# Token rows and gate sums of the channel mixing from y's high and low halves, behind the first receptance product

## Chip, cores and metric

One Trainium2 chip, one core. The time is the device time of the core in microseconds; the kernel before takes 770.95 us, the median of three runs (769.91 to 771.16).

## What is computed

Three layers one behind the other: attention under a block mask, channel mixing (RWKV's), and a mixture of eight experts in which a gate may hold the expert of the token before. The change lies in the second layer and in the hand-over to the third.

```python
def _moe_ref(x, mu_k, mu_r, w_k, w_v, w_r):          # x: 4 x 576 x 512
    x_prev = np.concatenate([np.zeros((B, 1, D)), x[:, :-1, :]], axis=1)
    xk = mu_k * x + (1.0 - mu_k) * x_prev
    xr = mu_r * x + (1.0 - mu_r) * x_prev
    k = np.maximum(xk @ w_k, 0.0)                    # 1024 wide
    v = k * k @ w_v
    r = 1.0 / (1.0 + np.exp(-(xr @ w_r)))
    return r * v                                     # called y below

def _moe2_ref(x, w_gate, w_local, w1, w2):           # x = y, token by token
    logits = x @ w_gate                              # 8 gates
    local_gate = 1.0 / (1.0 + np.exp(-(x @ w_local)))
    # the expert is argmax(logits) where local_gate < 0.5, else that of the token before
    # out = softmax(logits)[e] * (relu(x @ w1[e]) @ w2[e])
```

## The kernel before

All heavy products are done in two halves: an operand a is kept as its rounded part (type float32r, "hi") and the remainder ("lo"), and a product is hi*hi + hi*lo + lo*hi, three one-pass matmuls (`product`, lines 839 to 843). The high half is made by ACT with a copy, the low half by DVE with a subtraction.

The channel mixing takes the 2304 tokens in six steps of 384 columns (`NSTEP`, `NT`), features on the partitions. In step s the tensor engine (`mlp_step`, line 911) does eight K products of 12 matmuls (`k_done`), four receptance products R of 12 (`r_done`), then for s > 0 the rows of the step before (`rows_chunk(s - 1, c)`, four chunks), and four V products of 24 (`v_done`). V products use two PSUM banks in turn, so the third one waits for the first y: `wait(pe, y_done, DC * s + d - 1)`.

The rows: the third layer gathers tokens, so y (features on partitions, tile `yT`) is turned to token rows in DRAM, and the gate sums are made with it. `rows_chunk` multiplies 128 tokens of a chunk of yT, as the stationary operand, with 137 columns: the identity and beside it the nine gate columns of that chunk (tile `idw`). Both are plain float32. There are 12 such matmuls in a step. In the last step the rows of chunks 0 to 2 stand behind the V products 1 to 3, those of chunk 3 behind the loop (line 966).

ACT (`mlp_act`, line 1247) makes relu and the square's high half behind each K product, an exponential for each R product into tile `sig`, the high halves of the next step's inputs, and copies the rows from PSUM to `ytok` (`copy_rows`, three copies, after the logits are read). After the last step come the high halves of the first expert's weights (`split_we_hi`) and of its first token tile (`x_hi`).

DVE (`mlp_vec`, line 1536) makes the square and its low half for each K product, then for each exponential an addition and a reciprocal (lines 1562 and 1564), the low halves of the next step's inputs at the second and fourth, the gate sums of the step before (`read_logits`, three operations), and the four y (line 1578). In step 4 it routes the first twelve groups of tokens between the y (`pre_route`); PE takes part with small matmuls inside the V products (`between`). In step 5 it makes low halves of expert weights between the y (`first_weights`); after y 3 come the last rows, the last gate sums and the rest of the routing. SP stores `ytok` after the third copy and loads the first expert's weights in step 5; POOL gathers the token tiles.

Each engine runs its instructions in the order written; they wait for each other by semaphores with counts. PE's waits are written out by hand.

Of the kernel before, what the change touches and what calls it, by code (L numbers as in the profile page):

```python
# [5 lines left out]
F32 = mybir.dt.float32  # L6
# [4 lines left out]
ALU = mybir.AluOpType  # L11
# [5 lines left out]
def attention_moe_program(nc, qkT, v, mu_k, mu_r, w_k, w_v, w_r, w_gate9, w1, w2, out):  # L17
# [36 lines left out]
    with ExitStack() as ctx:  # L54
# [94 lines left out]
        yT = place("work", "yT", [P, DC, NT])  # L149
        ytok = place("work", "ytok", [P, GPS, DM])  # L150
        early_w2_raw = top["work"]
# [132 lines left out]
        def third_at(j):  # L284
# [8 lines left out]
                 "xm_split k_done relu_done ksq_done ksq_is_hi ksq_split r_done rexp_done sig_done v_done y_done "  # L293
# [5 lines left out]
         xm_is_hi, xm_split, k_done, relu_done, ksq_done, ksq_is_hi, ksq_split, r_done, rexp_done, sig_done, v_done, y_done,  # L299
# [63 lines left out]
        RW = P + GATE  # L363
# [326 lines left out]
        def _(pe):  # L690
# [133 lines left out]
            def rows_chunk(s, c):  # L824

                pe.wait_ge(y_done, DC * s + c + 1)
                at = PAD if c % 2 else PAD - GATE
                rhs = idw[:, c // 2, at:at + P + GATE]
                for g in range(GPS):
                    bank, col = (KB + g, c * RW) if c < DC - 1 else (KB + GPS, g * RW)  # L830
                    last = mm(ps[:, bank, col:col + RW], yT[:, c, g * G:(g + 1) * G], rhs, start=True, stop=True)  # L831
                return last
# [78 lines left out]
            def mlp_step(s):  # L911
# [27 lines left out]
                if s:  # L939
                    rows_free(s - 1)  # L940
                    for c in range(DC):
                        last = rows_chunk(s - 1, c)
                    last.then_inc(rows_done, 1)
# [205 lines left out]
        def _(act):  # L1149
# [97 lines left out]
            def mlp_act(s):  # L1247

                for f in range(FC):
                    k = FC * s + f  # L1250
                    act.wait_ge(k_done, k + 1)
                    wait(act, ksq_done, k - 1)
                    wait(act, ksq_is_hi, k - 1)
                    nc.scalar.activation(relu_k[:, f % 2, :], ps[:, KB + f % 2, 0:NT], ACT.Relu).then_inc(relu_done, 1)  # L1254
                    if s == 0:
                        xm_first(f // DC, 1 - f // DC, f % DC)
                    elif s + 1 < NSTEP:
                        xm_first(s + 1, f // DC, f % DC)
                    if s == 0 and f == DC:
                        xm_hi(0, 1)  # L1260
                    act.wait_ge(relu_done, k + 1)
                    nc.scalar.activation(ksq_hi[:, f, :], relu_k[:, f % 2, :], ACT.Square).then_inc(ksq_is_hi, 1)
                if s + 1 < NSTEP:
                    xm_hi(s + 1, 0)
                wait(act, y_done, DC * s)
                if s == 0:
                    act.wait_ge(norm_done, NHEAD)
                for d in range(DC):
                    act.wait_ge(r_done, DC * s + d + 1)
                    exp(sig[:, d, :], ps[:, RB + d % 2, 0:NT], scale=-1.0).then_inc(rexp_done, 1)  # L1270
                if s == 0:
                    for c in range(DC):
                        xm_first(1, 1, c)
                if s + 1 < NSTEP:
                    xm_hi(s + 1, 1)
                if s:
                    copy_rows(s - 1)

            def copy_rows(s):

                act.wait_ge(logits_read, s + 1)
                wait(act, y_stored, 16 * s)
                groups = ps[:, KB:KB + GPS, :]
                nc.scalar.activation(ytok[:, :, 0:2 * P], groups[:, :, GATE:GATE + 2 * P], ACT.Copy).then_inc(ytok_done, 1)
                nc.scalar.activation(ytok[:, :, 2 * P:3 * P], groups[:, :, 2 * RW + GATE:3 * RW],
                                     ACT.Copy).then_inc(ytok_done, 1)
# [33 lines left out]
            for s in range(NSTEP):  # L1320
                mlp_act(s)
            split_we_hi(0, 0)
            act.wait_ge(r_done, DC * NSTEP)
            act.wait_ge(ksq_split, FC * NSTEP)
            split_we_hi(0, 1)
            x_hi(0)
            copy_rows(NSTEP - 1)
# [41 lines left out]
        def _(dve):  # L1369
# [165 lines left out]

            def mlp_vec(s):
# [52 lines left out]
            def read_logits(s):  # L1589
# [5 lines left out]
                vec.tensor_reduce(lg, groups[:, :, 2 * RW - GATE:2 * RW + GATE].rearrange("p g (a e) -> p g e a", a=2),  # L1595
                                  AX.X, ALU.add).then_inc(lg_sums, 1)
                dve.wait_ge(lg_sums, 2 * s + 1)
# [317 lines left out]
```

## Time and profile before

| | |
|---|---|
| median of 3 runs | 770.95 us (769.91 to 771.16) |
| the profiled execution | 772.05 us, of it 770.3 in the span of instructions |
| mean granted clock of TensorE in it | 0.991 |
| attention | up to about 205 us of the span |
| channel mixing, steps 0 to 5 | 205 to 474 us, a step of 384 tokens about 45 us |
| routing and expert tiles | 474 to 770 us |

The profile is one execution. A row of the trace's timeline has a start from the beginning of the span, a duration, the engine, the source line, the operation with out<-in, the shapes and a count; behind it in brackets the idle time of the engine before it and what ended that. Successive matmuls overlap, so their cost is the distance of their starts, not their duration.

### The profile page before, as it was taken

How to read it: one execution, taken by the hardware profiler on the slowest of the kernel's cores; microseconds unless marked ns; L12 is line 12 of the kernel's file. 1: busy time of each engine (PE TensorE's matmuls, PEld its weight loads, DVE VectorE, ACT ScalarE, POOL GpSimd, SP SyncE). 2: the span in 40 equal slices, each digit the busy share in tenths (PEclk: the TensorE clock that was granted, in tenths of full speed). 3: DMA queues.
4: the chain of work that ended last, by engine and by line, in shares of the span. 5: the costliest groups of instructions: out<-in, count | busy, mean ns of one | idle time of the engine just before them, and what ended most of it. 6: DMA issues, size and time to landing. Idle time of an engine off the chain costs nothing.

```text
span 770.3 us, 13475 instructions
## 1 busy us (share of the span) xinstructions
PE 741.0 (96%) x4054; PEld 661.7 (86%) x4055; DVE 494.1 (64%) x905; ACT 357.5 (46%) x702; POOL 182.9 (24%) x215
## 2 busy tenths in 40 slices
PE   5999999998999999999999999999999999999994
PEld 4888888886989999999999998788888788888882
DVE  8899999996586856859487797622223745453261
ACT  4687877875652606244251432222124644353250
POOL 3345455453200000000020000223323232323231
PEclk9999999998999999999999999999999999999997
DMA  5667676551000010100101071167110176441000
GB/s 158 212 202 224 195 228 190 165 159 43 24 1 1 0 42 1 42 1 1 42 1 43 3 270 42 43 246 274 41 32 27 41 257 235 143 144 40 20 22 8
DMA packets 43063, 74.41 MB, mean 97 GB/s; under 512 B 10061, under 2 KB 20470, under 8 KB 43012
## 3 DMA queue, kind: packets, MB, share of 16 engines
q1 hardware_dynamic: 38676, 64.30, 25.3%
q0 software_dynamic: 4336, 9.47, 3.6%
q8 instruction: 27, 0.44, 0.2%
q14 instruction: 24, 0.20, 0.1%
HBM read 65.31 MB, written 10.57 MB: 99 GB/s over the span
## 4 chain that ended last, share of the span: by engine, by line
PE 83%; DVE 10%; issue 2%; ACT 2%; DMA 1%; ACTq 0%; POOL 0%; POOLq 0%; DVEq 0%
PE ps L841 20%; PE ps L842 20%; PE ps L843 20%; PE ps L779 3%; PE ps L707 2%; PE ps L999 2%; PE ps L733 2%; PE ps L732 2%; PE ps L831 2%; DVE negm L1380 2%; PE ps L710 2%; PE ps L774 1%; DVE sig L1564 1%; PE ps L753 1%; PE ps L908 1%
## 5 line engine op out<-in xcount | busy, mean ns | idle before, releaser
L841 PE MATMUL ps<-we_hi,hT_hi 128*128 (+1 forms) x176 | 73.4, 417 | 2.1 <-DVE o_sb L1856 1.4
L841 PE MATMUL ps<-we_hi,xgT_hi 128*128 (+1 forms) x176 | 70.6, 401 | 0.2 <-DVE xgT_lo L1755 0.2
L1317 ACT ACTIVATE hT_hi<-ps 128x512 fp32r<-128x512 f32 x44 | 26.1, 597 | 94.5 <-PE ps L999 49.4
L842 PE MATMUL ps<-we_lo,xgT_hi 128*128 (+1 forms) x176 | 69.7, 396 | 0.0
L843 PE MATMUL ps<-we_hi,xgT_lo 128*128 (+1 forms) x176 | 69.7, 396 | 0.0
L842 PE MATMUL ps<-we_lo,hT_hi 128*128 (+1 forms) x176 | 69.5, 395 | 0.0
L843 PE MATMUL ps<-we_hi,hT_lo 128*128 (+1 forms) x176 | 69.4, 394 | 0.0
L1151 ACT ACTIVATE pT<-ps 128x256 f32<-128x256 f32 (+2 forms) x192 | 63.1, 388 | 9.3 <-PE ps L733 8.9
L841 PE MATMUL ps<-xm_k_hi,wk_hi 128*128 128x384 f32 x192 | 65.2, 339 | 2.0 <-DVE ksq L1543 1.7
L841 PE MATMUL ps<-ksq_hi,wv_hi 128*128 128x384 f32 x192 | 66.0, 344 | 0.9 <-DVE yT L1578 0.9
L531 POOL TENSOR_TENSOR hi<-qk_raw,hi 64x576 fp32r<-64x576 f32 x32 | 45.2, 1412 | 85.8 <-DVE aug L1407 85.8
L842 PE MATMUL ps<-ksq_lo,wv_hi 128*128 128x384 f32 x192 | 64.9, 338 | 0.0
L843 PE MATMUL ps<-ksq_hi,wv_lo 128*128 128x384 f32 x192 | 64.9, 338 | 0.0
L843 PE MATMUL ps<-xm_k_hi,wk_lo 128*128 128x384 f32 x192 | 64.6, 336 | 0.0
L842 PE MATMUL ps<-xm_k_lo,wk_hi 128*128 128x384 f32 x192 | 64.5, 336 | 0.0
L1749 DVE TENSOR_TENSOR we_lo<-we_raw,we_hi (+1 forms) x48 | 55.6, 1221 | 11.3 <-ACT we_hi L1296 11.3
L1564 DVE RECIPROCAL sig<-sig 128x384 f32<-128x384 f32 x24 | 61.3, 2553 | 0.8
L1254 ACT ACTIVATE relu_k<-ps 128x384 f32<-128x384 f32 x48 | 23.6, 491 | 81.2 <-PE ps L843 81.2
L1762 DVE TENSOR_TENSOR hT_lo<-ps,hT_hi 128x512 fp32r<-128x512 f32 x44 | 30.0, 686 | 45.2 <-ACT hT_hi L1317 45.2
L1380 DVE TENSOR_REDUCE negm<-ps 128x1 fp32r<-128x128 f32 (+3 forms) x128 | 56.2, 479 | 2.1 <-PE ps L707 0.3
L732 PE MATMUL ps<-hi 128*128 128x256 f32 (+2 forms) x192 | 53.7, 297 | 2.3 <-ACT pT L1151 2.2
L628 POOL DMA_INDIRECT out<-o_sb,idx_out x21 | 21.5, 1023 | 139.4 <-DVE o_sb L1856 139.4
(277 smaller groups left out, 1835.4 us busy)
## 6 DMA issues: line engine op xcount, KB each, us to landing
we_raw<-w SPq DMA_DIRECT2D x12, 2048.0 KB, 11.8
qk_raw<-qkT SPq DMA_DIRECT2D x32, 576.0 KB, 3.9
v_sb<-v SPq DMA_DIRECT2D x16, 320.0 KB, 4.9
inv<-inv_scratch SPq DMA_DIRECT2D x32, 144.0 KB, 4.3
y_scratch<-ytok SPq DMA_DIRECT2D x6, 768.0 KB, 3.5
wk_raw<-w_k SPq DMA_DIRECT2D x8, 256.0 KB, 4.5
wv_raw<-w_v SPq DMA_DIRECT2D x8, 256.0 KB, 4.9
wr_raw<-w_r SPq DMA_DIRECT2D x4, 256.0 KB, 4.8
```

The costliest lines, as they stand in the source:

```text
L531: nc.gpsimd.tensor_tensor(hi[i % NBUF][DH:P, KEY, :], qk_raw[DH:P, i % 2, 1, :], hi[i % NBUF][DH:P, KEY, :].bitcast(F32), ALU.subtract).th ...
L732: mm(dst, hi[b][:, KEY, keys], hi[b][:, Q, q0:q1], start=True, stop=False)
L841: mm(dst, a_hi, b_hi, start=(k == 0), stop=False)
L842: mm(dst, a_hi, b_lo, start=False, stop=False)
L843: return mm(dst, a_lo, b_hi, start=False, stop=(k == n - 1))
L1151: return nc.scalar.activation(dst, src, ACT.Exp, **kw)
L1254: nc.scalar.activation(relu_k[:, f % 2, :], ps[:, KB + f % 2, 0:NT], ACT.Relu).then_inc(relu_done, 1)
L1317: nc.scalar.activation(hT_hi[:, half * FC // 2:(half + 1) * FC // 2, :].rearrange("p f t -> p (f t)"), ps[:, 3 + half, :], ACT.Copy).then_ ...
L1380: last = vec.tensor_reduce(negm[:, i % 2, t:t + 1], ps[:, bank, col:col + keys], AX.X, ALU.max, negate=True)
L1564: vec.reciprocal(sig[:, d, :], sig[:, d, :]).then_inc(sig_done, 1)
L1749: vec.tensor_tensor(we_lo[part][:, third], we_raw[part][:, third], we_hi[part][:, bass.ds(slot_at(j) + k * EPIECE, EPIECE)].bitcast(F32), ...
L1762: vec.tensor_tensor(hT_lo[:, fs, :].rearrange("p f t -> p (f t)"), ps[:, 3 + half, :], hT_hi[:, fs, :].rearrange("p f t -> p (f t)").bitca ...
```

## The change

- New tiles: `y_hi` and `y_lo`, of yT's size. `y_hi` lies where `sig` lies, `y_lo` where `yT` lies. `idr` holds the products' other operand in float32r: for each of two pairs of chunks the identity, with the high and the low part of nine gate columns on either side of it. It is made once, by five DVE operations after the last y of step 0 (`rows_rhs`).
- After each y (except chunk 3 of the last step) ACT makes `y_hi` (`cast_y`) and DVE `y_lo` (`split_y`), DVE waiting for ACT. In step 0 DVE makes all four low halves after y 3. In ACT's order the four casts of a step stand behind `copy_rows` of the step before; those of the last step stand before, between and behind the casts of expert weights.
- `rows_chunk` does two one-pass matmuls of 146 columns, y_hi and then y_lo by the same `idr`, added up in PSUM, in place of one float32 matmul of 137. Chunk 3 of the last step stays as it was.
- PE does the rows block of step s - 1 behind the first R product of step s, no longer behind the fourth.
- ACT waits for `rows_done` before the first exponential of a step.
- `read_logits` adds four gate parts in its first operation instead of two, and has five operations in place of three (four in the last step).

```diff
+        y_hi = nc.alloc_sbuf_tensor_at("y_hi", [P, DC, NT], R32, offset=top["work"] - 2 * 4 * DC * NT)
+        y_lo = nc.alloc_sbuf_tensor_at("y_lo", [P, DC, NT], R32, offset=top["work"] - 4 * DC * NT)
         ytok = place("work", "ytok", [P, GPS, DM])
+        idr = place("work", "idr", [P, 2, P + 4 * GATE], R32)
...
-        RW = P + GATE
+        RW = P + 2 * GATE
...
             def rows_chunk(s, c):
 
-                pe.wait_ge(y_done, DC * s + c + 1)
-                at = PAD if c % 2 else PAD - GATE
-                rhs = idw[:, c // 2, at:at + P + GATE]
+                if (s, c) == (NSTEP - 1, DC - 1):
+                    pe.wait_ge(y_done, DC * NSTEP)
+                    for g in range(GPS):
+                        last = mm(ps[:, KB + GPS, g * RW:g * RW + P + GATE], yT[:, c, g * G:(g + 1) * G],
+                                  idw[:, 1, PAD:PAD + P + GATE], start=True, stop=True)
+                    return last
+                pe.wait_ge(y_split, DC * s + c + 1)
+                at = 2 * GATE * (c % 2)
+                rhs = idr[:, c // 2, at:at + RW]
                 for g in range(GPS):
                     bank, col = (KB + g, c * RW) if c < DC - 1 else (KB + GPS, g * RW)
-                    last = mm(ps[:, bank, col:col + RW], yT[:, c, g * G:(g + 1) * G], rhs, start=True, stop=True)
+                    tokens = slice(g * G, (g + 1) * G)
+                    mm(ps[:, bank, col:col + RW], y_hi[:, c, tokens], rhs, start=True, stop=False)
+                    last = mm(ps[:, bank, col:col + RW], y_lo[:, c, tokens], rhs, start=False, stop=True)
                 return last
...
                     last.then_inc(r_done, 1)
-                if s:
-                    rows_free(s - 1)
-                    for c in range(DC):
-                        last = rows_chunk(s - 1, c)
-                    last.then_inc(rows_done, 1)
+                    if s and d == 0:
+                        pe.wait_ge(rhs_split, 2)
+                        rows_free(s - 1)
+                        for c in range(DC):
+                            last = rows_chunk(s - 1, c)
+                        last.then_inc(rows_done, 1)
...
                     act.wait_ge(norm_done, NHEAD)
+                wait(act, rows_done, s)
                 for d in range(DC):
                     act.wait_ge(r_done, DC * s + d + 1)
...
                 if s:
                     copy_rows(s - 1)
+                if s + 1 < NSTEP:
+                    for d in range(DC):
+                        cast_y(s, d)
+
+            def cast_y(s, d):
+
+                act.wait_ge(y_done, DC * s + d + 1)
+                nc.scalar.activation(y_hi[:, d, :], yT[:, d, :], ACT.Copy).then_inc(y_is_hi, 1)
...
             for s in range(NSTEP):
                 mlp_act(s)
+            cast_y(NSTEP - 1, 0)
             split_we_hi(0, 0)
+            cast_y(NSTEP - 1, 1)
             act.wait_ge(r_done, DC * NSTEP)
             act.wait_ge(ksq_split, FC * NSTEP)
             split_we_hi(0, 1)
             x_hi(0)
+            cast_y(NSTEP - 1, 2)
             copy_rows(NSTEP - 1)
...
+            def split_y(s, d):
+
+                dve.wait_ge(y_is_hi, DC * s + d + 1)
+                vec.tensor_tensor(y_lo[:, d, :], yT[:, d, :], y_hi[:, d, :].bitcast(F32), ALU.subtract).then_inc(y_split, 1)
+
+            def rows_rhs():
+
+                gates = [(idw[:, :, PAD - GATE:PAD], 0), (idw[:, :, PAD + P:PAD + P + GATE], 2 * GATE + P)]
+                vec.tensor_copy(idr[:, :, 2 * GATE:2 * GATE + P], idw[:, :, PAD:PAD + P])
+                for given, at in gates:
+                    vec.tensor_copy(idr[:, :, at:at + GATE], given).then_inc(rhs_hi, 1)
+                dve.wait_ge(rhs_hi, 2)
+                for given, at in gates:
+                    vec.tensor_tensor(idr[:, :, at + GATE:at + 2 * GATE], given, idr[:, :, at:at + GATE].bitcast(F32),
+                                      ALU.subtract).then_inc(rhs_split, 1)
...
                     vec.tensor_tensor(yT[:, d, :], ps[:, VB + d % 2, 0:NT], sig[:, d, :], ALU.mult).then_inc(y_done, 1)
+                    if s and (s + 1 < NSTEP or d + 1 < DC):
+                        split_y(s, d)
+                    if s == 0 and d == DC - 1:
+                        rows_rhs()
+                        for made in range(DC):
+                            split_y(0, made)
...
-                dve.wait_ge(lg_sums, 2 * s + 2)
-                vec.tensor_tensor(lg, lg, last_chunk[:, :, P:RW], ALU.add).then_inc(logits_read, 1)
+                dve.wait_ge(lg_sums, 4 * s + 2)
+                vec.tensor_tensor(lg, lg, groups[:, :, GATE:2 * GATE], ALU.add).then_inc(lg_sums, 1)
+                dve.wait_ge(lg_sums, 4 * s + 3)
+                if s + 1 < NSTEP:
+                    vec.tensor_tensor(lg, lg, last_chunk[:, :, P + GATE:RW], ALU.add).then_inc(lg_sums, 1)
+                    dve.wait_ge(lg_sums, 4 * s + 4)
+                vec.tensor_tensor(lg, lg, last_chunk[:, :, P:P + GATE], ALU.add).then_inc(logits_read, 1)
```

## Rows read from the trace of the kernel before

**Rows 1.** Page of the profile, busy time, share and instructions of each engine.
```profile
PE 741.0 (96%) x4054; PEld 661.7 (86%) x4055; DVE 494.1 (64%) x905; ACT 357.5 (46%) x702; POOL 182.9 (24%) x215
```

**Rows 2.** Timeline, rows block of step 1 (start, duration, engine, line, count).
```profile
267.56 2.96 PE L831 MATMUL ps<-idw,yT 128*128 128x137 f32 x24
...
270.28 0.43 PE L841 MATMUL ps<-ksq_hi,wv_hi 128*128 128x384 f32 x1
```

**Rows 3.** Timeline, one-pass matmuls with a new weight load each.
```profile
443.16 1.39 PE L882 MATMUL ps<-val,one_b_pre 128*128 128x2 f32 x12
...
481.80 1.01 PE L888 MATMUL ps<-val_pre,one_b_pre 128*128 128x144 f32 x8
```

**Rows 4.** Timeline of PE, step 1: end of the first R product, third V product.
```profile
261.15 0.33 PE L843 MATMUL ps<-xm_r_hi,wr_lo 128*128 128x384 f32 x1
...
278.85 0.34 PE L841 MATMUL ps<-ksq_hi,wv_hi 128*128 128x384 f32 x1
```

**Rows 5.** Timeline of ACT, step 1: a cast, the first exponential, the last rows copy.
```profile
260.33 0.51 ACT L1262 ACTIVATE ksq_hi<-relu_k 128x384 fp32r<-128x384 f32 x1
...
262.13 0.47 ACT L1151 ACTIVATE sig<-ps 128x384 f32<-128x384 f32 x1
...
278.92 0.50 ACT L1287 ACTIVATE ytok<-ps 128x384 f32<-128x384 f32 x1
```

**Rows 6.** Timeline of DVE, step 1: a low half, head and end of the chain.
```profile
261.01 0.55 DVE L1551 TENSOR_TENSOR ksq_lo<-ksq,ksq_hi 128x384 fp32r<-128x384 f32 x1
262.63 0.36 DVE L1562 TENSOR_SCALAR sig<-sig 128x384 f32<-128x384 f32 x1 [1.07 <-ACT sig L1151]
...
277.18 0.20 DVE L1595 TENSOR_REDUCE logits<-ps 128x27 f32<-128x54 f32 x1
277.41 0.18 DVE L1598 TENSOR_TENSOR logits<-logits,ps 128x27 f32<-128x27 f32 x1
277.63 0.18 DVE L1600 TENSOR_TENSOR logits<-logits,ps 128x27 f32<-128x27 f32 x1
277.73 0.55 DVE L1578 TENSOR_TENSOR yT<-ps,sig 128x384 f32<-128x384 f32 x1
```

**Rows 7.** Timeline of PE, step 0: third V product, with what it waited for.
```profile
234.16 0.45 PE L841 MATMUL ps<-ksq_hi,wv_hi 128*128 128x384 f32 x1 [0.93 <-DVE yT L1578]
```

**Rows 8.** Timeline of DVE and of PE, step 4: first y, routing, third V product.
```profile
413.10 0.55 DVE L1578 TENSOR_TENSOR yT<-ps,sig 128x384 f32<-128x384 f32 x1
...
415.57 0.17 DVE L1625 SCALAR_TENSOR_TENSOR fresh<-keep,a_of 128x12 f32<-128x12 f32 x1
...
414.10 0.34 PE L841 MATMUL ps<-ksq_hi,wv_hi 128*128 128x384 f32 x1
...
415.89 0.27 PE L848 MATMUL ps<-idw,fresh 128*12 128x128 f32 x1
```

**Rows 9.** Timeline of ACT, DVE and PE, step 5 and its end.
```profile
443.42 0.49 ACT L1151 ACTIVATE sig<-ps 128x384 f32<-128x384 f32 x1 [1.09 <-PE ps L843]
...
458.00 7.70 ACT L1296 ACTIVATE we_hi<-we_raw 128x1024 fp32r<-128x1024 f32 x8
...
458.56 0.55 DVE L1578 TENSOR_TENSOR yT<-ps,sig 128x384 f32<-128x384 f32 x1
...
468.11 3.49 DVE L1749 TENSOR_TENSOR we_lo<-we_raw,we_hi 128x1024 fp32r<-128x1024 f32 x3
472.49 0.56 DVE L1578 TENSOR_TENSOR yT<-ps,sig 128x384 f32<-128x384 f32 x1 [0.89 <-PE ps L843]
...
462.14 0.86 PE L831 MATMUL ps<-idw,yT 128*128 128x137 f32 x6
```

**Rows 10.** Windows: PE, PEld, DVE, ACT, POOL busy (count), PEclk, DMA share, GB/s.
```profile
182.20:185.60 3.40, 1.45 (x11) 1.01 (x9) 3.03 (x5) 1.52 (x4) 1.41 (x1) 1.00 0.02 3
185.60:192.40 6.80, 6.53 (x19) 5.18 (x20) 1.53 (x4) 3.72 (x10) 1.40 (x1) 0.50 0.10 24
...
211.00:214.50 3.50, 1.80 (x11) 1.48 (x10) 3.19 (x6) 3.25 (x9) 0.00 (x0) 1.00 0.00 0
```

More of the change, by code:

```diff
@@ L292, in attention_moe_program @@
                  "scores_t exp_done p_is_hi p_split v_split v_is_hi pv_done o_copied sums_chain norm_done wm_is_hi wm_split xm_tmp xm_summed xm_is_hi "
-                 "xm_split k_done relu_done ksq_done ksq_is_hi ksq_split r_done rexp_done sig_done v_done y_done "
+                 "xm_split k_done relu_done ksq_done ksq_is_hi ksq_split r_done rexp_done sig_done v_done y_done y_is_hi y_split rhs_hi rhs_split "
                  "rows_done lg_sums logits_read ytok_done chain pre_dve pre_pe first_known slot_0 slot_1 ranks_read rt_dve rt_pe rt_exp shifted p_known p_stored slots_known exps_known turns_known tables o_half "
@@ L298, in attention_moe_program @@
          scores_t, exp_done, p_is_hi, p_split, v_split, v_is_hi, pv_done, o_copied, sums_chain, norm_done, wm_is_hi, wm_split, xm_tmp, xm_summed,
-         xm_is_hi, xm_split, k_done, relu_done, ksq_done, ksq_is_hi, ksq_split, r_done, rexp_done, sig_done, v_done, y_done,
+         xm_is_hi, xm_split, k_done, relu_done, ksq_done, ksq_is_hi, ksq_split, r_done, rexp_done, sig_done, v_done, y_done, y_is_hi, y_split, rhs_hi, rhs_split,
          rows_done, lg_sums, logits_read, ytok_done, chain, pre_dve, pre_pe, first_known, slot_0, slot_1, ranks_read, rt_dve, rt_pe, rt_exp, shifted, p_known, p_stored, slots_known, exps_known, turns_known,
@@ L1283, in copy_rows @@
                 groups = ps[:, KB:KB + GPS, :]
-                nc.scalar.activation(ytok[:, :, 0:2 * P], groups[:, :, GATE:GATE + 2 * P], ACT.Copy).then_inc(ytok_done, 1)
-                nc.scalar.activation(ytok[:, :, 2 * P:3 * P], groups[:, :, 2 * RW + GATE:3 * RW],
+                nc.scalar.activation(ytok[:, :, 0:2 * P], groups[:, :, 2 * GATE:2 * RW - 2 * GATE], ACT.Copy).then_inc(ytok_done, 1)
+                nc.scalar.activation(ytok[:, :, 2 * P:3 * P], groups[:, :, 2 * RW + 2 * GATE:3 * RW],
                                      ACT.Copy).then_inc(ytok_done, 1)
@@ L1594, in read_logits @@
                 last_chunk = ps[:, KB + GPS, 0:GPS * RW].rearrange("p (g w) -> p g w", w=RW)
-                vec.tensor_reduce(lg, groups[:, :, 2 * RW - GATE:2 * RW + GATE].rearrange("p g (a e) -> p g e a", a=2),
+                vec.tensor_reduce(lg, groups[:, :, 2 * RW - 2 * GATE:2 * RW + 2 * GATE].rearrange("p g (a e) -> p g e a", a=4),
                                   AX.X, ALU.add).then_inc(lg_sums, 1)
-                dve.wait_ge(lg_sums, 2 * s + 1)
+                dve.wait_ge(lg_sums, 4 * s + 1)
                 vec.tensor_tensor(lg, lg, groups[:, :, 0:GATE], ALU.add).then_inc(lg_sums, 1)
-                dve.wait_ge(lg_sums, 2 * s + 2)
-                vec.tensor_tensor(lg, lg, last_chunk[:, :, P:RW], ALU.add).then_inc(logits_read, 1)
+                dve.wait_ge(lg_sums, 4 * s + 2)
[5 more added lines that the diff above has]
+                vec.tensor_tensor(lg, lg, last_chunk[:, :, P:P + GATE], ALU.add).then_inc(logits_read, 1)
             gate = logits[:, :, 0:NE].rearrange("p g e -> p e g")
```

## Prediction

> **What bounds the kernel now.** I read the busy line of the page first: PE is busy 96% of the span, DVE 64%, ACT 46% [rows 1]. Time can therefore leave only through PE work that is taken away, and any new PE wait is paid in full. So I looked next for what the rows block costs on PE, and then for which waits of PE hang on the vector engine in the channel mixing (205 to 474 us of the span). One such wait is already there: in step 0 the third V product starts 0.93 us late, because the first y of the step ended only just before [rows 7]. In steps 1 to 4 that y comes in time by little: in step 1 it runs from 277.73 for 0.55 us and the third V product starts at 278.85, 0.57 us behind its end [rows 4, 6]; in step 4 it is 413.65 against 414.10, 0.45 us [rows 8]; the steps between show the same pattern. Behind the last receptance product DVE runs a closed chain (add 1, reciprocal, the low halves, logits, y) without a gap, so whatever delays the chain's head delays this y by as much.
>
> **What the block of products costs.** Before, a full block is 24 PE records, each one matmul of two passes with its own weight load: 267.56 for 2.96 us, the next product at 270.28 [rows 2]. A record is 0.28 us long, so the pitch is (2.96 - 0.28) / 23 = 0.117 us. After, 12 products by y's high and 12 by y's low half are 24 matmuls and 24 weight loads again, of 146 columns in one pass. The nearest rows are one-pass matmuls with a new weight load each: 8 of 144 columns in 1.01 us, pitch (1.01 - 0.28) / 7 = 0.104; 12 of 2 columns in 1.39 us, pitch (1.39 - 0.25) / 11 = 0.104 [rows 3]. Two columns cost as much as 144: the load sets the pitch, and the number of loads does not fall. The bounds are thus a gain of 24 x 0.013 = 0.3 us a block and none; I take 0.15, five times, and 0.1 for the three small blocks of the last step: **-0.8 us**. The new block is then about 2.8 us long. The Trainium skill, TensorE: Matmul & The Clock Gate, section LDWEIGHTS, gives a load the number of its columns over 1.2 GHz, 107 ns for 128 columns; by that the gain would be 0.2 us a block, inside my bounds, and it speaks against hopes that fewer passes alone shorten this block.
>
> **What the move costs.** ACT now waits for all rows of the step before its first exponential, since y's high half lies where the exponential writes. The block starts when the first receptance product has been issued, 261.32 in step 1 (last matmul 261.15 plus one pitch of 0.17) [rows 4], and ends 2.8 us later, 264.1. The first exponential started at 262.13 [rows 5]; DVE followed at 262.63 and had waited 1.07 us for it [rows 6]. The head of the chain moves by 2.0 us. The sums over the gates get two more small operations of 0.22 us pitch and a longer reduction [rows 6]: 0.5. The first y of step 1 then ends at 278.28 + 2.5 = 280.8, and PE waits until 280.85 where it could have gone on at 278.7. Net of the cover of 0.5 us, **+2.0** in step 1, by the same sum **+1.9, +1.9 and +2.2** in steps 2 to 4. The cover is the gap between that y and the product; nothing else is late in its place, as PE waits for nothing between.
>
> The halves themselves: a cast on ACT is 0.51 us [rows 5], a subtraction on DVE 0.55 [rows 6], with hand-over 1.15 us that DVE spends behind each y. In steps 1 to 3 V products of 4.2 us cover it. For the first y the cast is queued behind the three copies of the rows, the last of which started 1.2 us after that y did [rows 5, 6]; so its low half ends 2.2 us after y. That is free in steps 1 to 3 (the next y is needed 4 us later). In step 0, five small operations of DVE for the operand (1.1 us, an estimate from the 0.2 us of its small operations in [rows 6]) and four subtractions (2.2) stand between the last y, which ends 0.6 us behind its product, and the first square of step 1, 0.55: 4.4 us, where PE has two K products (24 pitches of 0.175, 4.2 us) before it needs that square: **+0.1** (0 to 0.8).
>
> In **step 4** the routing of the first groups follows the first y on DVE, from the end of y at 413.65 to 415.74, and PE takes its result in the third V product at 415.89, 0.2 us after the nine matmuls ahead of it (414.10 + 1.6 = 415.7) [rows 8]. It now starts 2.2 us later behind y, while PE has the same 1.6 us of work: a second wait of 2.75 us, **+2.5** net. After the last y, the low half pushes the routing and the first square of step 5 by 1.15 us; PE's third K product waits for both: **+0.4**. The waits behind (local scan, counts) have 1 us or more to spare.
>
> In **step 5** nothing lies before the first exponential (443.42, idle 1.09 us before it) [rows 9], so it moves by the whole 2.6 us, and y of chunk 0 from 458.56 [rows 9] to 461.75, its end to 462.3. Cast and subtraction end at 463.45; PE wanted chunk 0's rows at 462.0 (462.14 before [rows 9]): a wait of 1.5. ACT has eight casts of expert weights (7.70 us) [rows 9] behind it, with y 1's cast between: to 471.1; the cast and subtraction of 512 columns for the first expert tile (0.6 and 0.7, estimates from the 384 columns of [rows 5, 6]) to 472.4; y 2 stands behind them on DVE, to 472.9, its low half to 474.0, then three subtractions of weights, 3.49 us [rows 9], to 477.4, and y 3 to 477.9. It ended at 473.05 before [rows 9], just behind its product. PE stands idle from 474.6 to 477.9. The routing chain that starts with y 3's rows moves by 4.8 us, and by 0.2 for the sums: **+5.0**. What ACT and DVE do here was hidden behind V products; that cover is used up. Sum of all: 0.1 + 2.0 + 1.9 + 1.9 + 2.2 + 2.5 + 0.4 + 5.0 = 16.0 us. The 0.8 us saved are not taken off again: in each of these steps DVE's chain ends PE's wait, and a shorter block shows only as an earlier exponential, which the 2.8 us has in it. SP's stores and POOL's first gather move along by 2 to 5 us and nobody is near waiting for them; after the routing the expert tiles are the same work.
>
> **The clock.** PE's granted clock was half (0.50, 1.2 of 2.4 GHz) over 185.6 to 192.4; just before, between 182.2 and 185.6, PE had stood idle 1.95 us. It stayed at 1.00 around 211 to 214.5, where PE idled 1.7 us [rows 10]. The new waits are 2.0 to 2.3 us in steps 1 to 4, in step 4 with a second one of 2.75 soon behind, and 3.3 us in step 5: the last two places idle most. A fall costs 6.6 us of work at half rate, 3.3 us where PE is the bound, and about 2.2 where the routing chain is. I take one in step 4 and one in step 5: +5.5. The bounds are 0 and five falls, 15.
>
> **Sum.** 16.0 + 5.5 = 21.5 us: the profiled execution's 772.05 becomes 793.6; that run lies 1.1 over the median of the three, so the forecast for the median is 770.95 + 21.5 = 792.5 us.
>
> **Rivals.**
> 1. The waits come, the clock holds: 787.0. For it: a pause of 1.7 us left the clock alone [rows 10], and the new ones are little longer. Chance 0.20.
> 2. The waits come and the clock falls at three or more further places: 770.95 + 16 + 11 = 798. Chance 0.10.
> 3. The covers hold, so it is not slower: the first y of a step would have to move by less than its slack of 0.45 to 0.6 us. For it: DVE is idle a third of the span. Against: its chain has no gap between exponential and y [rows 6], and ACT's new wait moves the head by 2 us. Then only the saving on PE is left: 770.95 - 0.8 = 770.2, no change. Chance 0.04.
> 4. Columns set the block's pitch, not loads: 146 columns at the pitch of 384 (0.17 [rows 4]) are 0.067 us, and the block takes 1.6 us, 1.2 less. The waits of steps 1 to 4 shrink by as much, and that of step 5's chain too: 770.95 + 16.0 - 6.0 = 781, with the clock held, and I say 782 for what of step 5 stays. The Trainium skill, same page, section Back-to-back issue gap, has a sustained 81 ns for a load with a 128-column matmul; by it the block would be 1.9 us and the time about 784. The rows of 144 and of 2 columns speak against both. Chance 0.05; together with rival 3 it would be faster, 764, chance 0.03.
> 5. A product of 146 columns is not done in one pass, but as before in two records: 48 records, the block 2.8 us longer in five steps: 770.95 + 16.0 + 14 to 17 = 801 to 804 with the clock held. Against: 8 products of 144 columns left 8 records [rows 3]. Chance 0.03.
>
> **How the numbers follow.** Forecast (waits and one to three falls) 0.55; the rivals as given. The range takes in rival 1, less 3 us for waits priced too high, and rival 2, plus the 0.8 us of doubt on step 0: 784 to 799; rivals 3 to 5 stay outside. Of the cases, 0.93 are slower, 0.04 the same, 0.03 faster; 0.2% is about what a measurement of this kernel can tell from no change.
>
> **What would show it.** Right: rows blocks of 24 one-pass records with a pitch of 0.10 to 0.115; the first exponential of a step right behind the block's end; PE idle about 2.1 us before the third V product in steps 1 to 4, released by DVE's y; 2.7 us before the transposition of the routing in step 4; y 3 of the last step 4 to 5 us behind its product; a granted clock of 0.5 for some 7 us in steps 4 and 5. Wrong: a third V product that starts on time (then the chain has slack I do not see), a block under 2 us (rival 4), or 48 records in it (rival 5). Weakest are the falls of the clock, 5.5 us of the 21.5, then the last step, where five queues' orders multiply.

## The result, and the profile after

| | before | after |
|---|---|---|
| median | 770.74 us (4 runs) | 788.12 us (4 runs, 787.76 to 791.58) |
| ratio to before | 1 | 1.0234 [1.0208, 1.0261] |
| the profiled execution, its span | 772.05, 770.3 us | 787.76, 786.0 us |
| mean granted clock in it | 0.991 | 0.989 |

The kernel is slower by 17.4 us in the medians, by 15.7 between the two profiled executions. From the page of the kernel after: the span, the busy time, the chain of work that ended last by engine, and the V products' group (count, busy, mean ns, idle before it and what ended that):

```profile
span 786.0 us, 13541 instructions
...
PE 742.4 (94%) x4054; PEld 660.9 (84%) x4055; DVE 508.3 (65%) x944; ACT 369.8 (47%) x725; POOL 182.3 (23%) x215
...
PE 74%; DVE 18%; ACT 3%; issue 2%; DMA 1%; ACTq 0%; POOL 0%; POOLq 0%; DVEq 0%
...
L852 PE MATMUL ps<-ksq_hi,wv_hi 128*128 128x384 f32 x192 | 66.4, 346 | 9.2 <-DVE yT L1618 9.2
```

PE has as many instructions as before, 4054, and is busy 742.4 us against 741.0 [rows 1]. All but 1.4 of the 15.7 us are therefore idle time of PE, and the last line names most of it: 9.2 us before V products, released by DVE's y. PE's waits by what ended them (total, times, longest) show the others. Of what these four rows hold, the kernel before has only 0.93 us, once [rows 7].

```profile
PE ps L852 <- DVE yT L1618: 9.2, 5, 2.2
...
PE ps L832 <- DVE yT L1618: 3.0, 1, 3.0
PE ps L859 <- DVE fresh L1676: 2.5, 1, 2.5
...
PE ps L841 <- DVE y_lo L1563: 1.4, 1, 1.4
```

In the order given: the third V product of steps 0 to 4, the rows of chunk 3 in the last step, the transposition of step 4's routing, the rows of chunk 0 in the last step. These are 16.1 us, and the first row holds the wait of step 0, which was there before.

**Step 1** on PE, after (timeline; start, duration, in brackets the idle time and what ended it):

```profile
259.30 0.34 PE L854 MATMUL ps<-xm_r_hi,wr_lo 128*128 128x384 f32 x1
259.47 0.23 PE L841 MATMUL ps<-idr,y_hi 128*128 128x146 f32 x1
259.54 0.28 PE L842 MATMUL ps<-idr,y_lo 128*128 128x146 f32 x1
259.65 0.28 PE L841 MATMUL ps<-idr,y_hi 128*128 128x146 f32 x1
...
261.99 0.28 PE L842 MATMUL ps<-idr,y_lo 128*128 128x146 f32 x1
262.11 0.39 PE L852 MATMUL ps<-xm_r_hi,wr_hi 128*128 128x384 f32 x1
...
279.06 0.45 PE L852 MATMUL ps<-ksq_hi,wv_hi 128*128 128x384 f32 x1 [2.18 <-DVE yT L1618]
```

The block is 24 records from 259.47 to 262.11, 2.64 us, where it took 2.72 from 267.56 to 270.28 [rows 2]: the pitch of its records is 0.11 us. It stands behind the first R product, and at 279.06 PE has idled 2.18 us. The same step on ACT, then on DVE:

```profile
262.36 0.49 ACT L1163 ACTIVATE sig<-ps 128x384 f32<-128x384 f32 x1 [1.98 <-PE ps L842]
264.44 0.49 ACT L1163 ACTIVATE sig<-ps 128x384 f32<-128x384 f32 x1 [1.59 <-PE ps L854]
...
279.65 0.50 ACT L1308 ACTIVATE ytok<-ps 128x384 f32<-128x384 f32 x1
280.02 0.54 ACT L1298 ACTIVATE y_hi<-yT 128x384 fp32r<-128x384 f32 x1
```

```profile
262.88 0.36 DVE L1602 TENSOR_SCALAR sig<-sig 128x384 f32<-128x384 f32 x1 [3.18 <-ACT sig L1163]
...
265.75 0.29 DVE L1602 TENSOR_SCALAR sig<-sig 128x384 f32<-128x384 f32 x1
...
277.42 0.26 DVE L1641 TENSOR_REDUCE logits<-ps 128x27 f32<-128x108 f32 x1
...
278.46 0.55 DVE L1618 TENSOR_TENSOR yT<-ps,sig 128x384 f32<-128x384 f32 x1
```

The first exponential waits for the block's last record (L842), and DVE has idled 3.18 us ahead of the addition against 1.07 [rows 6]. From the head of DVE's chain to its y is 15.58 us (262.88 to 278.46), where it was 15.10 (262.63 to 277.73 [rows 6]): 0.48 more, the longer sums. The chain has no other gap. The second exponential ends at 264.93, and DVE comes to it only at 265.75: in this kernel the head alone, and with it ACT's wait for the block, sets when y comes.

**Step 4**, DVE and then PE (first y, its low half, the routing's `fresh`, the transposition):

```profile
420.80 0.55 DVE L1618 TENSOR_TENSOR yT<-ps,sig 128x384 f32<-128x384 f32 x1
...
422.93 0.56 DVE L1563 TENSOR_TENSOR y_lo<-yT,y_hi 128x384 fp32r<-128x384 f32 x1 [1.58 <-ACT y_hi L1298]
...
425.38 0.17 DVE L1676 SCALAR_TENSOR_TENSOR fresh<-keep,a_of 128x12 f32<-128x12 f32 x1
```

```profile
425.70 0.27 PE L859 MATMUL ps<-idw,fresh 128*12 128x128 f32 x1 [2.47 <-DVE fresh L1676]
```

From the start of y to `fresh` DVE took 2.47 us before [rows 8] and takes 4.58: it waits 1.58 for ACT's cast, which stands behind the three copies of the rows, and then makes the low half.

**Step 5**, PE and then DVE:

```profile
473.68 0.31 PE L841 MATMUL ps<-idr,y_hi 128*128 128x146 f32 x1 [1.39 <-DVE y_lo L1563]
...
487.85 0.97 PE L832 MATMUL ps<-idw,yT 128*128 128x137 f32 x6 [2.98 <-DVE yT L1618]
```

```profile
471.85 0.55 DVE L1618 TENSOR_TENSOR yT<-ps,sig 128x384 f32<-128x384 f32 x1
...
483.36 0.56 DVE L1563 TENSOR_TENSOR y_lo<-yT,y_hi 128x384 fp32r<-128x384 f32 x1 [0.59 <-ACT y_hi L1298]
483.84 3.49 DVE L1800 TENSOR_TENSOR we_lo<-we_raw,we_hi 128x1024 fp32r<-128x1024 f32 x3
487.24 0.55 DVE L1618 TENSOR_TENSOR yT<-ps,sig 128x384 f32<-128x384 f32 x1
```

The last y stands behind the low half of the third y and three subtractions of weights, and PE idles 2.98 us for it. Before, it had been DVE that waited for PE there, 0.89 us [rows 9].

**The clock**: windows of the kernel after (length, busy us and count of PE, PEld, DVE, ACT, POOL, granted clock, DMA share, GB/s), around the third V product of steps 2 and 3, in step 4 and around the last rows:

```profile
323.20:326.70 3.50, 1.31 (x8) 0.99 (x7) 2.43 (x7) 1.36 (x3) 0.00 (x0) 1.00 0.00 0
370.00:373.20 3.20, 1.01 (x7) 0.69 (x6) 2.54 (x7) 0.95 (x2) 0.00 (x0) 1.00 0.00 0
373.30:376.60 3.30, 3.30 (x12) 3.30 (x11) 1.58 (x3) 1.46 (x4) 0.00 (x0) 0.50 0.59 230
418.00:425.70 7.70, 3.32 (x18) 2.71 (x17) 5.80 (x22) 1.99 (x4) 0.00 (x0) 1.00 0.27 103
484.50:489.30 4.80, 1.82 (x13) 1.59 (x12) 3.71 (x6) 0.00 (x0) 0.00 (x0) 1.00 0.00 0
489.40:492.60 3.20, 3.20 (x10) 2.33 (x9) 1.78 (x9) 1.57 (x3) 0.00 (x0) 0.50 0.09 35
```

In steps 1 to 3 PE does the same work around the same idle time, 2.18 or 2.19 us; the windows of steps 2 and 3 only cut it differently. The clock held behind the first two waits and fell to 0.50 (1.2 GHz) 0.5 us behind the third, for 3.4 us. In step 4, with two waits, it held; behind the last rows it fell again. Where it falls differs from one execution to the next: in the profiles of e3, e4 and e7 (below), whose steps 1 to 3 are those of this kernel, it fell at the end of the wait of step 2 or up to 0.5 us behind it, and not at step 3's.

**The account.** Lengths of the steps, from the start of the first K product to that of the next step's; the first of all starts at 197.64 us in the profile of before, so the channel mixing begins there and not at 205. e1 and e2 are experiments below: e1 moves the float32 block, e2 adds ACT's wait to it.

| step | before | e1 | e2 | after | after − before |
|---|---|---|---|---|---|
| 0 | 44.96 | 45.05 | | 45.08 | +0.12 |
| 1 | 44.73 | 45.94 | 46.43 | 46.75 | +2.02 |
| 2 | 45.08 | 45.70 | 46.43 | 46.91 | +1.83 |
| 3 | 45.09 | 45.71 | 46.43 | 48.44 | +3.35 (of it some 1.6 clock) |
| 4 | 46.30 | 47.37 | 48.12 | 50.76 | +4.46 |
| 5, to the last routing's transposition | 52.44 | | | 58.32 | +5.88 (of it some 0.7 clock) |

The clock's parts are differences too: from its third V product on, step 3 takes 10.11 us, steps 1 and 2 take 8.43 and 8.58, and I take 1.63 off; from chunk 3's rows to the transposition it is 4.08 us, in e3, e8 and e10, where no fall lies there, 3.41 or 3.42. The sum is 17.66 us. The profiled execution after entered the channel mixing 1.97 us earlier than that of before; with the 0.05 by which the tiles behind the routing differ that makes the 15.7 us between the two spans. In attention its clock was low for 3.4 us, not 6.8 [rows 10], which can be 1.7 of the 1.97 at most and need not be: e3, with 3.4 us too, entered at 197.54, only 0.1 earlier than before. Attention's code is the same in both kernels, so this part is not the change's.

### The profile page after: what moved, and what is told of

Its sections match the earlier page's. It is cut to its first block, busy times and chain, and to the rows that moved or that the text cites. A ratio compares the mean times of both kernels' runs of the same rounds, so it can differ in the third digit from the quotient of the medians.

```text
span 786.0 us, 13541 instructions
## 1 busy us (share of the span) xinstructions
PE 742.4 (94%) x4054; PEld 660.9 (84%) x4055; DVE 508.3 (65%) x944; ACT 369.8 (47%) x725; POOL 182.3 (23%) x215
## 4 chain that ended last, share of the span: by engine, by line
PE 74%; DVE 18%; ACT 3%; issue 2%; DMA 1%; ACTq 0%; POOL 0%; POOLq 0%; DVEq 0%
PE ps L852 17%; PE ps L854 17%; PE ps L853 17%; DVE sig L1604 6%; PE ps L782 3%; PE ps L710 3%; PE ps L736 2%; PE ps L735 2%; PE ps L1011 2%; DVE negm L1404 2%; PE ps L713 2%; PE ps L777 1%; PE ps L919 1%; DVE hi L1426 1%; DVE aug L1431 1%
## 5 line engine op out<-in xcount | busy, mean ns | idle before, releaser
L1806 DVE TENSOR_TENSOR xgT_lo<-ps,xgT_hi 128x512 fp32r<-128x512 f32 x23 | 15.8, 689 | 60.7 <-ACT xgT_hi L1323 58.8
```

## Experiments

My theory, T: the order alone makes DVE's chain late, since the block stands ahead of R products 2 to 4; ACT's wait adds to it, and the high and low halves lengthen the chain in steps 4 and 5. Rivals: W, ACT's wait is the whole cost of the move, as the prediction has it; H, the casts and subtractions of the halves cost by themselves; F, falls of the clock are a large part of the time. (The expectations call T theory A, W theory B and H theory C.) Every difference is between medians, to the kernel before measured beside the run; the ratio has its 95% interval.

| run | us | difference | ratio |
|---|---|---|---|
| e1, block moved, float32 | 776.69 | +4.97 | 1.0063 [1.0046, 1.0080] |
| e2, e1 and ACT's wait | 778.79 | +7.07 | 1.0089 [1.0068, 1.0110] |
| e3, after, routing first in step 4 | 789.39 | +17.67 | 1.0232 [1.0208, 1.0255] |
| e4, after, last step's rows float32 | 785.96 | +14.24 | 1.0176 [1.0157, 1.0195] |
| e5, halves, block in its old place | 771.32 | +0.47 | 1.0001 [0.9991, 1.0011] |
| e6, e5 with the block moved | 777.44 | +6.39 | 1.0084 [1.0065, 1.0102] |
| e7, e3 and e4 | 783.85 | +13.00 | 1.0163 [1.0139, 1.0186] |
| e8, after, waits filled | 787.82 | +16.97 | 1.0205 [1.0180, 1.0229] |
| e9, e5, step 0 in another order | 770.65 | −0.20 | 0.9992 [0.9982, 1.0003] |
| e10, e8 and e3's order | 783.98 | +12.93 | 1.0175 [1.0158, 1.0192] |

### e1 and e2: the order alone, and with ACT's wait

```diff
-                if s:
+                    if s and d == 0:
                         rows_free(s - 1)
...
+                wait(act, rows_done, s)      # e2 only
```

> The kernel before with one edit: the rows block (still float32, from yT) stands behind the first receptance product; ACT waits for nothing new. Theory A, the order alone costs: the first exponential stays where it is, but the second receptance product ends 2.8 us later, so DVE's second addition in steps 1 to 4 starts 1.25 to 1.5 us later than its place in the closed chain, and with 0.4 to 0.67 us of cover PE waits 0.85 to 0.9 us more before each third V product: 3.5 us; 0.4 more before the routing's transposition in step 4; step 5 moves by 1.1. Together +5.0: 775.7 us. Theory B, ACT's wait for the rows is the whole cost of the move: no change, 770.7. Theory C, the casts and subtractions of the halves are the cost: no change either.

> The first kernel of this group plus ACT's wait for rows_done before the first exponential; still float32, no halves. Theory A: the head of the chain moves by 2.05 to 2.25 us (the float32 block is 2.96 us long), net of the cover +1.7, +1.6, +1.6, +1.8 in steps 1 to 4, +0.4 in step 4's routing, step 5 +1.1 as without the wait: +8.2, 778.9 us. Theory B (the wait alone): 4 x 1.65 and what follows, 777 to 779, the same here, but then the kernel without the wait must be at 770.7. Theory C (the halves): 770.7. What is left to 788.1 is then the halves' part.

Measured: +4.97 and +7.07, where T had +5.0 and +8.2. PE's waits for y, e1 and then e2:

```profile
PE ps L841 <- DVE yT L1578: 3.7, 5, 0.7
```

```profile
PE ps L841 <- DVE yT L1579: 6.6, 5, 1.5
```

In e1 nothing but the place of the block differs from before, and its five waits of 0.7, in steps 0 to 4, stand where the kernel before has a single one, that of step 0. How they arise shows in step 1 of e1, on DVE and then on ACT:

```profile
262.38 2.55 DVE L1564 RECIPROCAL sig<-sig 128x384 f32<-128x384 f32 x1
...
266.36 0.36 DVE L1562 TENSOR_SCALAR sig<-sig 128x384 f32<-128x384 f32 x1 [1.43 <-ACT sig L1151]
```

```profile
261.48 0.47 ACT L1151 ACTIVATE sig<-ps 128x384 f32<-128x384 f32 x1
...
265.83 0.49 ACT L1151 ACTIVATE sig<-ps 128x384 f32<-128x384 f32 x1 [3.88 <-PE ps L843]
```

The first exponential starts 19.73 us behind the step's start, in the kernel before 19.53: the move hardly touches it. The second waits 3.88 us for PE, which does the block ahead of the second R product. DVE's reciprocal ends at 264.93 and DVE stands idle until 266.36: 1.43 us. Of 2.02, 1.83 and 1.72 us in steps 1 to 3 of the kernel after (the clock's part taken off), the order makes 1.21, 0.62 and 0.62 (e1 less before), ACT's wait 0.49, 0.73 and 0.72 (e2 less e1), the halves with their longer sums 0.32, 0.48 and 0.38. These are the shares when one is added to the other in this order. Once ACT's wait is there, it is what holds the chain, as step 1 of the kernel after shows. W falls as the whole cost: the wait adds 2.1 to make e2's 7.1 us, the order without it costs 5.0. T holds. (e1's profile also has one fall of the clock behind the routing, where its tiles take 1.56 us longer than before.)

### e5 and e6: the halves with a place of their own, late and early

`y_hi` lies in the place of `ytok`, so ACT need not wait; the low halves of y 0 to 2 are made behind y 2; steps 4 and 5 keep float32 rows. e6 differs from e5 in the place of the block alone.

```diff
+        y_hi = nc.alloc_sbuf_tensor_at("y_hi", [P, DC, NT], R32, offset=top["work"])
...
-                wait(act, rows_done, s)
...
+                wait(act, y_stored, 16 * s)          # ahead of cast_y
...
-                    if s and (s + 1 < NSTEP or d + 1 < DC):
-                        split_y(s, d)
+                    if s and s < NHALF and d >= 2:
+                        for made in range(DC - 1) if d == 2 else (DC - 1,):
+                            split_y(s, made)
...
-                if s:                                # e5
+                    if s and d == 0:                 # e6
```

> One-pass rows without the cost of their place: y's high half lies where the token rows (ytok) lie and not on the exponentials' tile, so ACT waits for no rows; the block stands behind the fourth receptance product as before; the low halves are made behind y 2 and y 3; steps 4 and 5 keep the float32 rows. Theory A (order and wait are the cost, the block itself gains little): the block is 2.63 us against 2.71, four times 0.1 to 0.15 us, less what the longer gate sums take out of the cover: 0.3 us under the kernel before, which a measurement hardly sees. Theory C (casts and subtractions cost by themselves): 3 us or more above it.

> One-pass rows, y's high half in the place of the token rows (so no wait of ACT for the rows), float32 rows for steps 4 and 5 as in the run with the block behind the fourth receptance product, but the block now stands behind the first, as in the change. Theory A (the order alone delays DVE's second addition): 1.2 us a step in steps 1 to 4, 0.4 at the routing, 1.1 in step 5: +6.2, 777.0 us. If only the shared place of y's high half and the exponentials were at fault: 771.3, as with the block behind the fourth.

Measured: +0.47, an interval that holds 1, and +6.39. PE in step 1 of e5, the block in its old place:

```profile
267.27 0.23 PE L844 MATMUL ps<-idr,y_hi 128*128 128x146 f32 x1
...
269.80 0.28 PE L845 MATMUL ps<-idr,y_lo 128*128 128x146 f32 x1
269.91 0.39 PE L855 MATMUL ps<-ksq_hi,wv_hi 128*128 128x384 f32 x1
```

The one-pass block is 2.64 us, 0.08 shorter than the float32 one [rows 2]; four of them would be 0.3 us, which these runs can't tell from nothing. So H falls where V products cover the casts and low halves: they cost nothing that can be measured there, and the new products gain nothing that can be. In e5's profile steps 1 to 3 are together 0.26 us shorter than before and step 4 is 0.58 longer. There PE waits 0.43 us ahead of the transposition, where it did not before. The waits for y, e5 and then e6, show what the early place does to the same instructions:

```profile
PE ps L855 <- DVE yT L1619: 1.0, 2, 0.7
```

```profile
PE ps L855 <- DVE yT L1619: 6.3, 5, 1.5
```

### e4: the last step's rows in float32

The edit gives all rows of the last step the branch that chunk 3 has, with 137 columns, and leaves their casts and low halves out.

```diff
-                if (s, c) == (NSTEP - 1, DC - 1):
+                if s >= NHALF:                       # NHALF = 5
...
-            cast_y(NSTEP - 1, 0)
             split_we_hi(0, 0)
-            cast_y(NSTEP - 1, 1)
...
-            cast_y(NSTEP - 1, 2)
```

> The changed kernel with the rows of the last step all in float32 as before, and so without casts and low halves of the last step's y. If those set the wait before the rows of chunk 0 and the lateness of y 3 (4.7 us in step 5), what is left of step 5 is about 1.5 us, from the late chain alone: -3.2, 784.9 us. If step 5 is late only because its exponentials are, the time stays at 788.1.

Measured: +14.24, 3.1 us less than the kernel after has (+17.38). PE's idle time ahead of chunk 0's rows went from 1.39 to 0.24 us, that ahead of chunk 3's from 2.98 to 0.79. Step 5 is 54.11 us long up to the last transposition, against 58.32 (of it 0.7 clock) after and 52.44 before. So some 3.5 of the last step's 5.2 us are the halves' own; the rest is the late head of the chain, which is not the halves': e1, float32 throughout, has 0.86 of idle time at chunk 3 and a step 5 of 53.42. In this step H holds.

### e3, e7, e8 and e10: step 4's routing, and the clock

e3 puts the routing ahead of the low halves in step 4; e7 is e3 and e4 together.

```diff
-                    if s and (s + 1 < NSTEP or d + 1 < DC):
+                    if s and s != NSTEP - 2 and (s + 1 < NSTEP or d + 1 < DC):
                         split_y(s, d)
...
                     if s == NSTEP - 2:
                         pre_route(d)
+                        split_y(s, d)
```

> The changed kernel with one order turned on DVE in step 4 only: the low half of y d is made behind the routing's part d, not ahead of it. If the second wait of step 4 (PE before the routing's transposition) comes from the cast and subtraction queued ahead of the routing, it shrinks from 2.6 us to about 0.5: -2.1, 786.0 us. If it comes from the late y itself, nothing changes: 788.1.

> The changed kernel with both repairs: the low halves of step 4 behind the routing, and the last step's rows in float32. If the parts add up (2.3 us for step 4's order, 3.2 for step 5) what is left is the late chain in five steps, 9.4 us above the kernel before, plus 0 to 3 us for falls of the clock: 780.5 to 784 us. If step 4's order is worth nothing, as the time of the run with it alone suggests, 785 to 786, as with the last step alone.

Measured: e3 +17.67, no less than the kernel after, where 2.1 us less was expected. The wait of 2.5 before step 4's transposition is gone in its profile. But the clock fell three times in the channel mixing there, against once before the last rows in the kernel after. The third of these falls, windows of e3:

```profile
448.00:451.40 3.40, 3.40 (x21) 3.40 (x21) 3.30 (x8) 2.03 (x4) 0.00 (x0) 1.00 0.00 0
451.40:454.80 3.40, 3.40 (x24) 3.40 (x23) 2.62 (x7) 1.02 (x2) 0.00 (x0) 1.00 0.29 60
454.80:457.90 3.10, 3.10 (x30) 3.10 (x30) 0.38 (x2) 0.49 (x1) 0.00 (x0) 1.00 0.98 394
457.90:461.30 3.40, 3.40 (x13) 3.40 (x13) 2.53 (x1) 0.00 (x0) 0.00 (x0) 0.50 0.99 383
```

At half clock 3.4 us do the work of 1.7, so three falls are 5 us at most, an estimate, which would hide the gain; that is arithmetic on one profile and not yet a proof. e7 gave +13.00, 1.2 us less than e4, and its step 4 is 48.74 us long, 2.02 less than after's 50.76. To settle it, e8 keeps PE at work in the waits: products of 512 columns, whose result nobody reads (9 in each of steps 1 to 4, 10 before the transposition, 6 and 12 before chunks 0 and 3 of the last step). e10 is e8 with e3's order and without the ten.

```diff
+                for _ in range(n):
+                    mm(ps[:, 3, :].rearrange("p (a q) -> p a q", a=4), ident_r[:, :], fill_ident, start=True, stop=True)
...
+                    if s and s < NSTEP - 1 and d == 2:
+                        pe.wait_ge(rexp_done, DC * s + DC)
+                        fill(9)
```

> The changed kernel with products of 512 columns that nobody reads (0.22 us each) put on PE where its trace shows it waiting: 9 ahead of the third V product in steps 1 to 4, 10 ahead of the routing's transposition in step 4, 6 and 12 ahead of the rows of chunks 0 and 3 in step 5, all shorter than the waits. If the waits let the clock fall and that costs time, the clock stays at 1.00 from 200 us on and the time drops by the falls' cost, 2 to 4 us: 784 to 786. If the falls cost nothing (the engine waits in them anyhow), 788.

> The changed kernel with the waits filled (products nobody reads, so that the clock doesn't fall there) and, in step 4, the low halves behind the routing; nothing is filled in ahead of the transposition, where the wait should be gone. Against the filled kernel without that order (17.0 us above the kernel before) the queue theory says 2.2 us less: 14.8 above, 785.6. If the order is worth nothing: 787.8.

Windows over the channel mixing, the kernel after and then e8:

```profile
200.00:489.00 289.00, 271.30 (x1588) 267.32 (x1587) 213.25 (x354) 122.26 (x235) 8.40 (x29) 0.99 0.08 30
```

```profile
200.00:490.00 290.00, 287.08 (x1664) 280.16 (x1663) 215.35 (x359) 123.16 (x238) 8.54 (x29) 1.00 0.08 31
```

PE is busy 287 of 290 us in e8 and the clock does not fall there; its profile has one fall later, at 495.6, behind the last transposition. The time came down by only 0.4 us (16.97 against 17.38), where I had expected 2 to 4. Steps 1 to 4 of e8 are 46.91, 47.15, 46.99 and 50.48 us, 191.5 together, and those of the kernel after without its fall 191.2. So filling takes the fall in step 3 away and gives 0.3 back; against the kernel after little is won: most of what PE's idle time costs, it costs filled as well. e10 gave +12.93, 4.0 us less than e8. Its step 4 is 48.51 us against 50.48: 1.97 us are the routing's order, as in e7. Between the two profiled executions, 5.2 us apart, another 1.6 lies behind the last transposition (295.50 us in e8, with its fall, 293.89 in e10, whose clock fell nowhere between attention and the end) and 0.95 ahead of the channel mixing.

e10 has a second comparison in it: it differs from e3 by the filled waits alone, and it is 4.7 us faster (12.93 against 17.67; the intervals of the ratios lie apart). Windows over the channel mixing, e3 and then e10:

```profile
200.00:491.00 291.00, 275.84 (x1598) 272.37 (x1596) 214.29 (x355) 123.49 (x238) 8.66 (x29) 0.98 0.08 31
```

```profile
200.00:487.00 287.00, 283.61 (x1652) 277.24 (x1651) 214.61 (x361) 122.80 (x237) 8.73 (x29) 1.00 0.08 31
```

The steps of e3 in which its clock fell, 2, 4 and 5, are 48.55, 49.49 and 58.92 us, those of e10 46.91, 48.51 and 57.37: 1.6, 1.0 and 1.6 us, 4.2 together. The mean granted clock over the four executions was 0.986 in e3, 0.989 in the kernel after, 0.993 in e8 and in e10. So the clock took e3's gain: its falls cost 4.2 us in the profile where those of the kernel after cost 2.3, and the order in itself is worth 2.0 us in step 4, as e7 and e10 show. F falls as an account of the change, 2.3 of 17.66 us in the kernel after; but between two variants falls can hide a gain of 2 us. Why e3 falls more often than the kernel after is not shown.

### e9: step 0

On e5, the low half of step 1's K input is made behind the first y of step 0, not ahead of it.

```diff
-                    if s + 1 < NSTEP and (d == 1 or s and d == DC - 1):
+                    if s and s + 1 < NSTEP and d in (1, DC - 1):
                         xm_lo(s + 1, d // 2)
...
+                    if s == 0 and d == 0:
+                        xm_lo(1, 0)
```

> The same, and in step 0 DVE makes the low half of the next step's K input behind the first y and not between the second and third reciprocal. PE's wait of 0.9 to 1.1 us before the third V product of step 0, which the kernel before has too, should go: 1.2 us under the kernel before in all, 0.9 us under the run without it. If another engine is late there, the same time as without it.

Measured: −0.20 to before, 0.9992 [0.9982, 1.0003], and 0.67 less than e5. In its profile PE no longer waits for y in step 0, and the step is 44.10 us long, against 44.96. 0.9 us on a step are seen, 0.2 to 0.7 in the whole, where 1.2 under the kernel before was expected; it is the fastest variant here and can't be told from the kernel before.

## Why the prediction was right, and where it was not

The forecast was 792.5 us (784 to 799), slower with a chance of 0.93; the kernel takes 788.1. The result lies between the forecast and rival 1 (787.0, the waits without falls), nearer to the rival.

| step of the sum | forecast | measured |
|---|---|---|
| step 0 | +0.1 | +0.12 |
| steps 1, 2, 3 | +2.0, +1.9, +1.9 | +2.02, +1.83, +1.72 |
| step 4, both waits | +2.2 + 2.5 | +4.46 |
| step 5 with its first square | +0.4 + 5.0 | +5.2 |
| waits together | 16.0 | 15.35 |
| falls of the clock | 5.5 | 2.3 (one execution) |

**The block.** Expected 2.8 us long with a pitch of 0.10 to 0.115; it is 2.64, pitch 0.11. That the number of columns does not set the pitch held (0.104 us for 2 and for 144 columns [rows 3]), and rivals 4 and 5 (a block under 2 us, 48 records) fell. That it is the weight load which sets it fits, but no run varies the load alone. The gain of 0.15 a block was 0.08. The Trainium skill, TensorE: Matmul & The Clock Gate, section LDWEIGHTS, gives a load the number of its columns over 1.2 GHz, 107 ns for 128 columns; the measured pitch of 111 ns (259.54 to 261.99 in step 1, 22 distances) agrees with it within 4%. The 81 ns of its section Back-to-back issue gap is seen in no rows block of these runs.

**Steps 1 to 3.** The sums fit within 0.2 us, and so does the working: PE idles 2.18 us before the third V product where 2.1 was expected, and from the first exponential to y DVE's chain has no gap. What the working does not say is how near the next limit lies, for it follows the first exponential alone. The second one is late too and comes 0.8 us before DVE wants it. Without ACT's wait the order alone therefore still makes 2.45 of the 5.57 us (e1: DVE idle for 1.43 us ahead of its second addition); ACT's wait adds 1.94, the halves 1.18. A reader who had drawn from the prediction the remedy "give y_hi a place of its own" would have won only a part: e6 does that, its steps 1 to 3 are still 3.8 us longer than before, and it is 6.4 us slower in all, although its last two steps have float32 rows.

**Step 4** went as worked out: 4.58 us from y to `fresh`, 2.1 more than before, and PE idle for 2.47 where 2.75 was expected. Taking the low half out of the way brought 2.0 us (e7, e10), not 2.5.

**Step 5.** Chunk 0's rows wait 1.4 us (1.5), y 3 ends 54.18 us behind the step's start (433.61 to 487.79), before 49.26 (423.79 to 473.05): 4.9 us later, as forecast (4.8). It was the term with the most steps in it and the one feared weakest after the clock. Y 3, and chunk 3's rows with it, came behind a low half and three subtractions of weights, as it had in its working.

**The clock** is the term that was mis-sized: 5.5 us against 2.3. Two falls came in the stage, the number taken, but one in step 3 instead of step 4, and each lasted 3.4 us and cost 1.6 and 0.7, where 3.3 and 2.2 had been taken from a single stretch of 6.8 us [rows 10] (half of it is 3.4). No row shows the 2.2. One stretch was too little to draw a length from. That the number came out is luck: in e3, e4 and e7, whose steps 1 to 3 are the same, the first fall came in step 2, e3 had three in the channel mixing, and e4 one in step 4 that did last 6.8 us (its step 4, with the code of the kernel after, is 51.99 us against 50.76).

**Covers** (rival 3) fell: no third V product of steps 0 to 4 started on time.

## What to carry to other kernels

Moving a block of work of the bounding engine costs what stands behind it there, not only what the moved work waits for: follow each event that the next engine's chain takes (here four exponentials, not the first alone), compare it with when that chain is ready for it, and ask which one holds the chain when the first is out of the way. Where a chain feeds the bounding engine with half a microsecond of slack, as here DVE's from exponential to y, what enters it is paid once the slack is used up: 0.5 us of longer sums cost 0.3 to 0.5 us a step behind the moved block and next to nothing with the block in its old place. Twenty-four one-pass products with a weight load each (2.64 us) were hardly cheaper than twelve of two passes (2.72). An operation that only a later stage needs (here the low halves) belongs behind what the next instruction of the bounding engine waits for. And a variant that shows no gain in its time may have won it where the clock took it back: compare the lengths of single steps, with and without a fall.

## What the runs showed of the hardware

- Apart from the stretch in which each kernel ends, a stretch at half clock lasted 3.4 or 6.8 us. In attention it was 6.8 in the profiles of before, e4 and e5 and 3.4 in the others, at the same place of the program; in the channel mixing it was 6.8 once, in step 4 of e4.
- The same work did not always have the same effect. At PE's idle time of 1.91 to 2.19 us before the third V product the clock held in step 1 every time; it fell at its end, or within 0.8 us, in step 3 (after), in step 2 (e3, e4, e7) and in step 4 (e3, e4). In e3 it also fell at 457.9 although PE had been busy without a gap for the 9.9 us before, of these the last 3.8 with 24 products of 146 columns and then twelve of 2 columns. Idle time ahead is thus not the only thing that comes before a fall.
- Products that nobody reads, put into the waits, kept the clock at 1.00 over the channel mixing. They won 0.4 us against the kernel after, within what these runs can tell, and 4.7 us against e3.
